# Output rows of a DMA-bound kernel: GpSimd's queue and its two row DMAs taken out, their rows put on SP

## The chip, the cores and the metric

The kernel runs on one core of one Trainium2 chip. Time is device microseconds of one execution, a median over several. The core has five engines: PE (TensorE), DVE (VectorE), ACT (ScalarE), POOL (GpSimd) and SP (SyncE), and 16 DMA engines that move data between HBM and the on-chip memory.
## The reference

Linear attention, then a soft mixture of experts, in float32:

```python
kv  = einsum('bhsd,bhse->bhde', k, v)                 # batch 8, heads 8, seq 576, dim 64
out = einsum('bhsd,bhde->bhse', q, kv)
x   = out / sqrt(mean(out*out, -1) + 1e-6) * g_norm   # -> 4608 tokens x 512
logits = x @ phi                                      # 4608 x 32 slots, 8 experts x 4 slots
d   = softmax of logits over the tokens               # 4608 x 32
slot_input = d.T @ x                                  # 32 x 512
slot_out[e] = relu(slot_input[e] @ w1[e]) @ w2[e]     # w1 8 x 512 x 1024, w2 8 x 1024 x 512
c   = softmax of logits over the slots
y   = c @ slot_out                                    # 4608 x 512
```

Read are q, k, v and the two weight tensors, 61.9 MB; written is y, 9.4 MB.

## The kernel before, in words

All large arrays pass through one on-chip buffer, `arena`, of 128 partitions (rows). SP issues nearly every transfer, and the order of its instructions is the order in which the DMA engines get work: first q, k and v by batch, then the weights in the rows of `W_ROWS`, each load as soon as its place in the arena is free, and at the end the output. The kernel keeps its own list of operations (`Order`), works out the waits of each from what it reads and writes (`settle`), and issues them at one line (`emit`, line 214, the waits at 213); this is why all rows of the profile have line 214. After the last operation SP waits at line 227 for every DMA that nobody has waited for.

The computation runs in stages of two token tiles (products, squares, root, logits, running maxima and sums), then the experts (`expert_h`, `expert_y`), and last the output. The output is made in 12 chunks, n = 0 to 11. A chunk is 128 rows of `CHUNK` = 1536 floats (6 KB a row, 768 KB in all). `output(hf, k, f)` makes chunk n: four matmuls, one ACT copy and one DVE copy from PSUM into the arena. Chunks 0 to 5 belong to the first half of the columns (hf = 0), 6 to 11 to the second; between the two PE has the rest of `expert_y` for the second half.

Chunks 3 to 11 are stored with three DMAs of all 128 rows by SP: chunks (3,4,5), (6,7) and (8,9,10,11) (`OUT_ROWS`), each issued once its last chunk has been copied. A DMA over 128 rows gives each DMA engine the same 8 rows.

Chunks 0, 1 and 2 are stored otherwise, by `store_first(n)`, which walks the list `FIRST`. Each entry is one DMA: an issuing engine, the first row `p0`, the step between rows, the number of rows `n`, the size `a` of the outermost dimension of the destination, the number of parts `c` into which each row is cut, and the chunks `k0` to `k1` that it takes of every row. It is issued after chunk `k1 - 1`:

```python
FIRST = (
    ("sync", 1, 4, 30, 5, 1, 0, 1), ("sync", 121, 4, 2, 3, 3, 0, 1),
    ("gpsimd", 1, 4, 24, 2, 1, 1, 2), ("gpsimd", 97, 4, 8, 2, 1, 1, 2),
    ("sync", 3, 4, 32, 1, 1, 0, 2), ("sync", 0, 2, 64, 1, 1, 0, 3), ("sync", 1, 2, 64, 1, 1, 2, 3),
)
STEPS = (7, 6)
```

The destination is written as `a` groups, and piece number j goes to group j mod a. So 30 rows with a = 5 go in five groups of six rows. `first_pieces` undoes this order on the host. `step_over(m)` issues a DMA of m tiny pieces from POOL, which carries nothing that is used (16 bytes per piece, from an input to the tile `stepped`). It is called once ahead of the experts with 7, and once between the two GpSimd entries of `FIRST` with 6.

Of the kernel before, what the change touches and what calls it, by code (L numbers as in the profile page):

```python
# [5 lines left out]
F32 = mybir.dt.float32  # L6
# [5 lines left out]
P = 128  # L12
# [41 lines left out]
OUT_ROWS = ((0, 1, 2), (3, 4, 5), (6, 7), (8, 9, 10, 11))  # L54
CHUNK = 4 * 12 * 32
FIRST = (
    ("sync", 1, 4, 30, 5, 1, 0, 1), ("sync", 121, 4, 2, 3, 3, 0, 1),
    ("gpsimd", 1, 4, 24, 2, 1, 1, 2), ("gpsimd", 97, 4, 8, 2, 1, 1, 2),
    ("sync", 3, 4, 32, 1, 1, 0, 2), ("sync", 0, 2, 64, 1, 1, 0, 3), ("sync", 1, 2, 64, 1, 1, 2, 3),
)  # L60
STEPS = (7, 6)
SHARED = (5, 11)
HEAD = 144
SCRATCH = 1024
# [210 lines left out]
def first_pieces(out):  # L275

    at = 0
    for _, p0, step, n, a, c, k0, k1 in FIRST:
        size = (k1 - k0) * CHUNK
        part = out[at : at + n * size]  # L280
        rows = part.reshape(n * c // a, a, size // c).swapaxes(0, 1)
        yield p0, step, n, k0, k1, rows.reshape(n, size)
        at += n * size

def soft_moe_linear_attention(nc, first_in, kv_in, q0_in, q1_in, kv4_in, kv5_in, t3_in, w_in, out):

    const = Const(nc)
# [9 lines left out]
    def place(at, n):  # L299
        return arena[:, HEAD + at * KB : HEAD + at * KB + n]  # L300
# [64 lines left out]
    nc.gpsimd.memset(ones, 1.0)  # L365
    zeros = const.tile([P, 256], BF16, name="zeros")
    nc.vector.memset(zeros, 0.0)
    stepped = const.tile([P, 16], F32, name="stepped")
    small = const.tile([P, 4], F32, name="small")
    eps = small[:, :1]  # L370
    nc.gpsimd.memset(eps, EPS_RMS)
# [304 lines left out]
    ends = {starts[s + 1] - 1: s for s in range(len(STAGES))}  # L676
# [194 lines left out]
    def expert_h(e):  # L871
        ph = ps.tile([P, 2, 512], F32, tag="m", name=f"ph{e}")[:, 0, :256]
        for c in range(4):
            for j in range(4):
                nc.tensor.matmul(
                    ph[32 * j : 32 * j + 32],
                    lhsT=sTe[:, (4 * e + c) * NS : (4 * e + c + 1) * NS],
                    rhs=w_block("w1", e, 4 * c + j),
                    start=c == 0,
                    stop=c == 3,  # L880
                )
        h = wk.tile([P, 256], F32, tag="part", name=f"h{e}", bufs=3)
        nc.scalar.activation(h, ph, AF.Relu, scale=rs)

        x = xts[(NT - 1 - e // 2) % NX].rearrange("p j n -> p (j n)")
        hTs[e] = x[:, e % 2 * 256 : e % 2 * 256 + 256].rearrange("p (c n) -> p c n", n=NS)
        nc.vector.transpose(out=hTs[e].rearrange("p c n -> p (c n)"), in_=h)
# [31 lines left out]
            nc.tensor.matmul(pz[f], lhsT=sel.rearrange("p a n -> p (a n)"), rhs=ys[hf][f], start=True, stop=True)  # L919
        zs[hf] = halves(f"z{hf}", pz)  # L920

    def step_over(n):
        ends = [x[:n, : 2 * w].rearrange("p (c n) -> p c n", c=2)[:, :, :4] for x, w in ((stepped, 8), (first_in, 64))]
        nc.gpsimd.dma_start(*ends)

    steps = list(STEPS[::-1])

    def store_first(n):
        at = 0
        for engine, p0, step, m, a, c, k0, k1 in FIRST:  # L930
            size = (k1 - k0) * CHUNK
            if k1 == n + 1:
                src = place(OUT_AT[k0], size)[p0 : p0 + step * (m - 1) + 1 : step]
                dst = out[:, at : at + m * size]
                if c > 1:
                    src = src.rearrange("p (c n) -> p c n", c=c)
                dst = dst.rearrange("o (b a n) -> (o a) b n", a=a, n=size // c)
                getattr(nc, engine).dma_start(dst, src)
                if engine == "gpsimd" and steps:
                    step_over(steps.pop())  # L940
            at += m * size

    def output(hf, k, f):
# [29 lines left out]
        if n <= OUT_ROWS[0][-1]:  # L973
            store_first(n)
        for row in OUT_ROWS[1:]:
            if row[-1] == n:
# [2 lines left out]
                    out[:, lo * P : (lo + m) * P].rearrange("o (p n) -> (o p) n", p=P), place(OUT_AT[row[0]], m)  # L979
                )  # L980

    step_over(steps.pop())
    expert_h(0)
    load_w("w2", 3)
    expert_h(1)
# [33 lines left out]
def build_program():  # L1019
    import concourse.bacc as bacc  # L1020

    nc = bacc.Bacc("TRN2", target_bir_lowering=False, num_devices=1, dynamic_dma_scratch_size=SCRATCH)
    shapes = {
        "first": (P, HEAD + 2304), "kv": (4, P, TOK), "q0": (P, TOK), "q1": (P, 2048),
        "kv4": (P, 2560 + TOK), "kv5": (P, 2 * TOK), "t3": (P, 3 * TOK),
        "w": (1, 2 * NE * P * UNIT),
    }
    args = [nc.dram_tensor(f"in_{n}_dram", s, F32, kind="ExternalInput").ap() for n, s in shapes.items()]
    args.append(nc.dram_tensor("out_0_dram", (1, 4 * NCH * P * 4 * CT * NS), F32, kind="ExternalOutput").ap())
    order = Order(nc)  # L1030
    soft_moe_linear_attention(order, *args)
    order.emit()
    return nc
# [61 lines left out]
```

How the kernel before makes its waits and increments, by code:

```python
    def emit(self):  # L203
        nc = self.nc
        counters = {e: nc.alloc_semaphore(f"done_{e}") for e in ENGINES[:4]}
        sems = list(counters.values())
        counts = dict.fromkeys(counters, 0)
        for op in self.ops:
            method, args, kwargs = op.call
            engine = getattr(nc, op.engine)
            *before, last = sorted(op.waits, key=lambda w: w.i) or [None]
            for w in before:
                engine.wait_ge(w.sem, w.value)
            inst = getattr(engine, method)(*args, **kwargs)
            if last is not None:
                inst.wait_op(last.sem, last.value, "sem-ge")
            if op.dma:
                op.sem, op.value = nc.alloc_semaphore(f"dma_{op.i}"), 16
                sems.append(op.sem)
                inst.then_inc(op.sem, 16)
            elif op.signals:
                counts[op.engine] += 1
                op.sem, op.value = counters[op.engine], counts[op.engine]
                inst.then_inc(op.sem, 1)
        for op in self.ops:
            if op.dma and not op.signals:
                nc.sync.wait_ge(op.sem, 16)
        numbers = sorted(s.num for s in sems)
        assert numbers == list(range(numbers[0], numbers[-1] + 1))
        nc.sync.sem_clear(range(numbers[0], numbers[-1] + 1))
```

## Time and profile before

| What | Value |
|---|---|
| time, median of 3 runs (lowest, highest) | 172.08 us (171.82 to 172.19) |
| profiled execution, its own time | 171.97 us |
| its span, first to last instruction | 170.6 us |
| bytes moved by the DMA engines | 71.65 MB, mean 420 GB/s |
| busy share of the span: PE, PEld, DVE, ACT, POOL | 87%, 62%, 51%, 52%, 35% |
| DMA packets: SP's queue (q1), GpSimd's queue (q0) | 3994, 352 |

The page cuts the span into 40 slices; its row DMA gives the mean busy share of the 16 DMA engines in tenths, its row GB/s what they moved. The view of DMA queues gives the same for any stretch, with the packets that start in it.
### The profile page before, as it was taken

What the parts mean: (1) busy time and instruction counts of PE and PEld (TensorE: products, weight loads), DVE (VectorE), ACT (ScalarE), POOL (GpSimd) and SP (SyncE); (2) the same over time, 40 slices, a digit from 0 to 9 for tenths busy, and PEclk for the clock granted to TensorE, in tenths of its full rate; (3) what the DMA queues carried; (4) which work ended last, traced back from release to release, by engine and by line L of the source; (5) the groups of instructions that cost most, each with busy time, mean ns of one, the idle gap of its engine ahead of it and who ended that gap; (6) DMA issues with size and microseconds to landing.
All of it is one profiled execution on the core that took longest, in us unless ns stands there. A gap on an engine that the chain in (4) does not pass through costs nothing.

```text
span 170.6 us, 4233 instructions
## 1 busy us (share of the span) xinstructions
PE 149.0 (87%) x1832; PEld 105.0 (62%) x1832; DVE 86.6 (51%) x185; ACT 89.0 (52%) x230; POOL 59.6 (35%) x73
## 2 busy tenths in 40 slices
PE   7989696989999899999899998989999989989300
PEld 3468576979778888897697674346655543455000
DVE  1122156284677266762946698823888137218400
ACT  3027576796975886859759864202223045217400
POOL 7000707648357745377382679500000004000000
PEclk9999999999999999999999999999999999999955
DMA  5999999999999999999999999999999999999996
GB/s 186 417 429 421 444 415 439 473 416 452 462 415 421 432 441 430 419 399 451 415 449 407 455 392 421 447 434 415 430 426 442 436 442 392 431 419 434 416 455 277
DMA packets 4365, 71.65 MB, mean 420 GB/s; under 512 B 790, under 2 KB 790, under 8 KB 922
## 3 DMA queue, kind: packets, MB, share of 16 engines
q1 hardware_dynamic: 3994, 71.18, 97.8%
q8 instruction: 14, 0.23, 0.5%
q0 software_dynamic: 352, 0.20, 0.4%
q14 instruction: 5, 0.04, 0.1%
HBM read 61.94 MB, written 9.44 MB: 418 GB/s over the span
## 4 chain that ended last, share of the span: by engine, by line
PE 58%; DMA 13%; ACT 12%; DVE 7%; SPq 2%; issue 1%
PE psum L214 58%; DMA arena<-in_kv_dram 13%; ACT bd L214 3%; ACT sq L214 3%; ACT xall L214 2%; SPq L214 2%; DVE arena L214 1%; DVE logits L214 1%; ACT arena L214 1%; DVE ms L214 1%; ACT part L214 1%; ACT d L214 1%; DVE part L214 1%; ACT r L214 1%; DVE acc L214 1%
## 5 line engine op out<-in xcount | busy, mean ns | idle before, releaser
L214 PE MATMUL psum<-bd,arena 128*128 128x192 f32 (+1 forms) x320 | 56.1, 335 | 1.9 <-ACT bd L214 1.5
L214 PEld LDWEIGHTS psum<-bd,arena 128*128 128x128 f32 (+1 forms) x320 | 45.4, 179 | 8.7 <-ACT bd L214 2.8
L214 DVE TENSOR_REDUCE ms<-sq 128x16 f32<-128x1024 f32 (+1 forms) x19 | 22.1, 1162 | 32.8 <-ACT sq L214 32.5
L214 POOL TENSOR_TENSOR part<-part,r 128x512 f32<-128x512 f32 x17 | 17.8, 1048 | 49.6 <-DVE r L214 49.6
L214 POOL TENSOR_TENSOR xall<-xall,r 128x512 f32<-128x512 f32 x34 | 34.7, 1042 | 0.0
L214 ACT ACTIVATE sq<-psum 128x512 f32<-128x512 f32 x36 | 21.5, 598 | 11.7 <-PE psum L214 11.2
L214 PE MATMUL psum<-arena 128*64 128x64 f32 (+1 forms) x640 | 21.7, 226 | 2.8 <-DMA arena<-in_kv_dram 2.7
L214 PEld LDWEIGHTS psum<-arena 128*64 128x64 f32 (+1 forms) x640 | 19.0, 137 | 8.2 <-DMA arena<-in_kv_dram 3.6
L214 ACT COPY xall<-psum 128x512 f32<-128x512 f32 x34 | 20.6, 606 | 0.0
L214 ACT COPY part<-psum 128x256 f32<-128x256 f32 (+1 forms) x38 | 13.6, 359 | 11.2 <-DVE part L214 10.0
L214 DVE TENSOR_REDUCE logits<-part 128x64 f32<-128x512 f32 (+1 forms) x18 | 17.8, 988 | 0.0
L214 PE MATMUL psum<-logits,part 32*128 32x384 f32 x96 | 13.5, 523 | 1.5 <-ACT arena L214 0.7
L214 PE MATMUL psum<-arena,xall 128*32 128x256 f32 x256 | 14.7, 380 | 0.0
L214 ACT COPY arena<-psum 128x768 f32<-128x768 f32 (+1 forms) x14 | 10.2, 754 | 5.3 <-PE psum L214 5.2
L214 POOL DMA_DIRECT2D out_dram<-arena x2 | 1.2, 589 | 33.4 <-ACT arena L214 33.4
L214 PE MATMUL psum<-arena,sq 128*32 128x256 f32 x224 | 12.7, 379 | 0.2 <-DVE sq L214 0.2
L214 DVE COPY arena<-psum 128x768 f32<-128x768 f32 (+1 forms) x12 | 10.3, 888 | 4.7 <-PE psum L214 4.7
L214 PEld LDWEIGHTS psum<-arena,xall 128*32 128x32 f32 x256 | 8.3, 110 | 6.0 <-issue 1.0
L214 PE MATMUL psum<-xall,d 128*32 128x258 f32 x144 | 10.8, 390 | 0.8 <-ACT d L214 0.8
L214 PEld LDWEIGHTS psum<-logits,part 32*128 32x128 f32 x96 | 6.3, 183 | 7.8 <-ACT arena L214 4.3
L214 ACT COPY bd<-psum 64x128 f32<-64x128 f32 (+1 forms) x32 | 9.9, 309 | 1.6 <-PE psum L214 1.4
L214 PEld LDWEIGHTS psum<-arena,sq 128*32 128x32 f32 x224 | 7.2, 110 | 5.1 <-DVE sq L214 0.5
(80 smaller groups left out, 124.1 us busy)
## 6 DMA issues: line engine op xcount, KB each, us to landing
arena<-in_w_dram SPq DMA_DIRECT2D x4, 4096.0 KB, 23.5
arena<-in_w_dram SPq DMA_DIRECT2D x4, 2048.0 KB, 20.0
arena<-in_t_dram SPq DMA_DIRECT2D x1, 6912.0 KB, 36.1
arena<-in_w_dram SPq DMA_DIRECT2D x2, 3072.0 KB, 22.6
arena<-in_kv_dram SPq DMA_DIRECT2D x2, 2304.0 KB, 23.6
arena<-in_kv_dram SPq DMA_DIRECT2D x1, 4608.0 KB, 42.8
arena<-in_kv_dram SPq DMA_DIRECT2D x1, 3584.0 KB, 32.4
arena<-in_kv_dram SPq DMA_DIRECT2D x3, 1152.0 KB, 12.0
```

Of the source, the lines that this page charges most:

```text
L214: inst = getattr(engine, method)(*args, **kwargs)
```

## The change

`FIRST` loses the column of the issuing engine: all entries are issued by SP. The two GpSimd entries, which stored rows 1, 5, 9, ... of chunk 1, are gone, and so are `step_over`, `STEPS` and the tile `stepped`. Those rows of chunk 1 now go with the last entry, which takes all odd rows of chunks 1 and 2 (it took chunk 2's alone). Rows 3, 7, ... are now stored for chunk 0 alone in their entry (before: chunks 0 and 1), and that entry is issued after chunk 0. Rows 1, 5, ... of chunk 0 are split anew: 25 rows in five groups, and 7 rows, each cut in two parts, in two groups. The number of SP's store DMAs stays five for these chunks.

```diff
 FIRST = (
-    ("sync", 1, 4, 30, 5, 1, 0, 1), ("sync", 121, 4, 2, 3, 3, 0, 1),
-    ("gpsimd", 1, 4, 24, 2, 1, 1, 2), ("gpsimd", 97, 4, 8, 2, 1, 1, 2),
-    ("sync", 3, 4, 32, 1, 1, 0, 2), ("sync", 0, 2, 64, 1, 1, 0, 3), ("sync", 1, 2, 64, 1, 1, 2, 3),
+    (1, 4, 25, 5, 1, 0, 1), (101, 4, 7, 2, 2, 0, 1), (3, 4, 32, 1, 1, 0, 1),
+    (0, 2, 64, 1, 1, 0, 3), (1, 2, 64, 1, 1, 1, 3),
 )
-STEPS = (7, 6)
...
-    stepped = const.tile([P, 16], F32, name="stepped")
...
-    def step_over(n):
-        ends = [x[:n, : 2 * w].rearrange("p (c n) -> p c n", c=2)[:, :, :4] for x, w in ((stepped, 8), (first_in, 64))]
-        nc.gpsimd.dma_start(*ends)
-
-    steps = list(STEPS[::-1])
-
     def store_first(n):
         at = 0
-        for engine, p0, step, m, a, c, k0, k1 in FIRST:
+        for p0, step, m, a, c, k0, k1 in FIRST:
...
-                getattr(nc, engine).dma_start(dst, src)
-                if engine == "gpsimd" and steps:
-                    step_over(steps.pop())
+                nc.sync.dma_start(dst, src)
...
-    step_over(steps.pop())
     expert_h(0)
```

## Rows read from the trace of the kernel before

**Rows 1.** The page: DMA busy share and rate in 40 slices, and the queues.
```profile
DMA  5999999999999999999999999999999999999996
GB/s 186 417 429 421 444 415 439 473 416 452 462 415 421 432 441 430 419 399 451 415 449 407 455 392 421 447 434 415 430 426 442 436 442 392 431 419 434 416 455 277
...
q1 hardware_dynamic: 3994, 71.18, 97.8%
...
q0 software_dynamic: 352, 0.20, 0.4%
```

**Rows 2.** Windows: busy time of each engine, PE's clock, DMA share and GB/s.
```profile
20.00:136.00 116.00, 110.85 (x1418) 82.68 (x1422) 71.14 (x156) 70.27 (x194) 52.68 (x54) 1.00 1.01 431
136.00:146.00 10.00, 8.66 (x70) 4.15 (x60) 5.59 (x8) 5.23 (x8) 1.72 (x3) 1.00 0.99 420
146.00:158.00 12.00, 11.26 (x144) 6.38 (x145) 4.31 (x7) 4.17 (x8) 0.00 (x0) 1.00 1.01 421
```

**Rows 3.** Timeline from 159 us on: start, duration, instruction.
```profile
159.68 0.48 ACT L214 COPY arena<-psum 128x384 f32<-128x384 f32 x1 [0.34 <-PE psum L214]
160.27 0.33 SPq L214 DMA_DIRECT2D out_dram<-arena  x1
```

**Rows 4.** SP's waits from 136 us on: in total, times, longest.
```profile
SPq L227 <- DMA out_dram<-arena: 9.6, 2, 7.2
```

**Rows 5.** DMA queues, 168.4 to 169.2 us: packets that start there, by size.
```profile
DMA packets 15, 0.25 MB, mean 307 GB/s; under 512 B 5, under 2 KB 5, under 8 KB 5
```

**Rows 6.** DMA queues, 169.2 to 169.8 us.
```profile
DMA packets 2, 0.02 MB, mean 41 GB/s; under 512 B 1, under 2 KB 1, under 8 KB 1
```

**Rows 7.** 169.8 to 170.0 and 170.0 to 170.2 us: 40 slices of 5 ns.
```profile
GB/s 0 1 0 0 0 1 0 0 0 0 0 0 0 0 0 0 0 0 0 0 0 0 0 0 0 0 0 0 0 0 0 0 1 0 0 0 0 1 1 0
DMA packets 5, 0.00 MB, mean 0 GB/s; under 512 B 5, under 2 KB 5, under 8 KB 5
...
GB/s 0 0 0 0 0 0 1 0 0 0 0 1 0 0 1 0 1 0 0 0 0 0 0 0 0 1 0 0 0 0 0 0 0 0 0 0 0 0 0 0
```

**Rows 8.** DMA queues, 146 to 158 us: packets, MB, share of the 16 engines.
```profile
DMA packets 733, 5.06 MB, mean 421 GB/s; under 512 B 356, under 2 KB 356, under 8 KB 486
...
q1 hardware_dynamic: 415, 4.84, 95.1%
q0 software_dynamic: 317, 0.20, 5.6%
```

**Rows 9.** DMA queues, 143.5 to 145.6 us, and 145.6 to 146.0 us.
```profile
DMA packets 56, 0.84 MB, mean 398 GB/s; under 512 B 5, under 2 KB 5, under 8 KB 5
...
DMA packets 19, 0.22 MB, mean 553 GB/s; under 512 B 4, under 2 KB 4, under 8 KB 6
```

**Rows 10.** Instructions that store the output, 138-142, 142-144, 143-145 and 145-161 us.
```profile
L214 SPq DMA_DIRECT2D out_dram<-arena x3: 530/722/951, 140.2 to 142.0; - x3
...
L214 POOL DMA_DIRECT2D out_dram<-arena x2: 569/589/609, 142.2 to 143.4; - x2
...
L214 SPq DMA_DIRECT2D out_dram<-arena x2: 502/546/589, 142.8 to 143.3; - x2
...
L214 SPq DMA_DIRECT2D out_dram<-arena x3: 332/344/358, 147.2 to 160.3; - x3
```

**Rows 11.** The page's DMA issues: count, KB each, us from issue to landing.
```profile
out_dram<-arena SPq DMA_DIRECT2D x1, 3072.0 KB, 10.2
...
out_dram<-arena SPq DMA_DIRECT2D x2, 384.0 KB, 9.7
out_dram<-arena POOLq DMA_DIRECT2D x1, 144.0 KB, 11.9
out_dram<-arena POOLq DMA_DIRECT2D x1, 48.0 KB, 15.4
```

More of the change, by code:

```diff
@@ L277, in first_pieces @@
     at = 0
-    for _, p0, step, n, a, c, k0, k1 in FIRST:
+    for p0, step, n, a, c, k0, k1 in FIRST:
         size = (k1 - k0) * CHUNK
```

## The prediction

> **What bounds the kernel now.** I read the page first, its DMA rows before its engines. The 16 DMA engines are full in every slice but the first and the last, and SP's queue alone fills 97.8% of them [rows 1]. The windows say the same: 431 GB/s from 20 to 136 us, 420 and 421 in the two stretches behind [rows 2]. PE is busy too, but it isn't what ends last: the last copy starts at 159.68 us, SP issues the last store at 160.27 [rows 3], and from there to the end no compute engine does anything, while SP waits for stores, 9.6 us in two waits [rows 4]. The last store has 3072 KB and lands 10.2 us after its issue [rows 11], at 160.27 + 10.2 = 170.5 of a span of 170.6. At 431 GB/s it would need 7.3 us by itself, so it stands behind other work: the DMA engines are behind the computation by some 3 us. The computation could be earlier or a little later and the end would not move. What sets the end is the DMA engine with the most to carry, and how evenly the bytes lie over the 16.
>
> Then I cut the end into narrow windows and counted the 4-byte packets, one per DMA engine, with which the last store ends. Five engines close it before 169.2 us [rows 5], one between 169.2 and 169.8 [rows 6], five in 169.8 to 170.0 and five in 170.0 to 170.2 [rows 7]. A slice there is 5 ns, and the 1s are the packets: the first of these ten is at 169.805 us, the third at 169.96, the last at 170.125 (SP sees it some 0.35 us later). So ten of 16 engines end within 0.32 us, and the other six up to 1.7 us earlier. Any change that leaves the sum of bytes alone can gain only what those six have spare; it loses as soon as one of the last ten gets more.
>
> **The change part by part.** One DMA engine carries 431 / 16 = 26.9 GB/s [rows 2], so 6 KB (one row of one chunk) is 0.228 us and 12 KB is 0.456 us.
>
> *Which engine gets what.* The bytes that move are rows 1, 5, ... of chunks 0 and 1, 384 KB. I deal them out by the code: a piece goes to group j mod a, and I take a group for one DMA engine.
>
> Before: 36 KB to each of engines 0 to 4 (30 rows in five groups); two more rows, 12 KB, which I take for engine 0, since the source has 2 rows and the destination 3 groups, with no count in common; over GpSimd 72 KB to each of two engines (24 rows in two groups) and 24 KB to each of two (8 rows). The counts 7, 2, 6, 2 of GpSimd's four DMAs add up to 17, one more than 16; if they are dealt in turn from engine 0, the pairs are 7 and 8, and 15 and 0. Engine 0 then has 36 + 12 + 24 = 72 KB, engines 1 to 4 have 36, 7 and 8 have 72, 15 has 24, and eight engines have nothing: 72 + 144 + 144 + 24 = 384.
>
> After: 30 KB to each of engines 0 to 4 (25 rows), 42 KB to engine 0 (7 rows against 2 groups, again no common count), and chunk 1's rows spread evenly, 12 KB each. Engine 0 has 84, engines 1 to 4 have 42, the other eleven 12: 84 + 168 + 132 = 384.
>
> The difference: +12 KB (+0.456 us) for nine engines (0 and the eight that had nothing), +6 KB (+0.228) for four, -12 KB for one, -60 KB (2.3 us) for two. The two will end early, and nothing uses their time.
>
> *What the nine do to the end.* Only six engines close before 169.8 us [rows 5, 6]. So at least three of the nine are among the last ten, which gives a new end no earlier than that of the third of the ten. The lower bound is therefore 169.96 + 0.456 = 170.42, 0.29 us behind 170.125 [rows 7], the upper one 0.456 us. Nine engines out of 16 will nearly always hold one of the last five, so I take the upper end, +0.45. If GpSimd's pairs lie elsewhere, at least 16 - 5 - 4 = 7 engines have nothing before and 12 KB after, against six early ones: the argument stands.
>
> The Trainium skill (DMA: Bandwidth & Descriptors, "Why a DMA increments its semaphore by 16 and not by 1") says that the engines used are the largest number up to 16 that divides the slowest dimension of both sides, the lowest-numbered from SP, and in turn from GpSimd; by that rule the shares are as I dealt them. No row of before names a DMA engine.
>
> *GpSimd's queue goes away.* From 146 to 158 us its 317 packets take 5.6% of the 16 engines [rows 8], 0.67 us on each. The 192 KB that it carried are 12 KB per engine, 0.456 us, and are still carried by SP's queue. The rest, 0.67 - 0.456 = 0.21 us per engine, is some 285 tiny packets, 18 per engine, and is saved. Outside the packets the queue might slow the others. The bound above: the rate is 421 GB/s there against 431 before, over 12 us that is 0.28 us in all; but it is 420 from 136 to 146 [rows 2], where that queue carries nothing yet (its first two packets start behind 145.6 us, as do the first rows of 6 KB [rows 9]), so I count the packets' 0.21 alone. The bound below is nothing, if other tiny packets take their place.
>
> *Smaller pieces.* Engine 0 gets 14 pieces of 3 KB for six of 2 KB. A tiny packet costs 0.21 / 18 = 12 ns, so eight more are at most 0.1 us, on that engine alone. I count nothing, since the other eight set the same end.
>
> *Issues on SP.* It issues five DMAs for these chunks before and after, 502 to 951 ns each [rows 10]. One moves from chunk 1 to chunk 0, GpSimd's two vanish, and chunk 1's rows now wait for chunk 2. The last issue of before starts at 143.3 us [rows 10], and the first row of 6 KB leaves behind 145.6 [rows 9]. So every store of these chunks is in the queue some 2 us before an engine comes to it, and the order costs nothing. Without that cover each late issue would cost its 0.5 us. Behind them SP has nothing until 147.2 [rows 10]. POOL has nothing to do there, and the two tiny copies signal nobody. The two engines that lose 60 KB come to the last store 2.3 us earlier, at about its issue; a wait there costs nothing, since they have that time spare.
>
> *Sum.* +0.45 - 0.21 = +0.24 us on the profiled execution's 171.97, so 172.21. The median shown is 0.11 above that execution, so 172.08 + 0.24 = **172.32 us**, 0.14% slower. Differences below 0.2%, 0.34 us, are about what a measurement of this kernel can't tell from nothing. The case's own range goes from +0.29 - 0.28 to +0.46, and 0.1 for engine 0: 172.09 to 172.64.
>
> **The rivals.**
>
> *Engine 0 is overloaded (slower).* If GpSimd's second pair does not hold engine 0, this engine goes from 48 to 84 KB: 36 KB, 1.37 us. Should it be one of the last ten, the end moves by 1.37 - 0.21 = 1.16 us, to 173.2. If instead the two-group DMA does use two engines, 21 KB each, engines 0 and 1 go from about 40 to 63 KB, 0.87 us, and the end by 0.66, to 172.7. For it: nothing in the entries evens engine 0 out. Against it: before, engine 0 has 48 KB from SP alone and may be one of the six early ones. It decides if engine 0 ends now after 170.12 + 0.45 - 1.37 = 169.2 us.
>
> *The two terms cancel (no change).* The last engines are mainly the four with +0.23, and the saving is 0.28: -0.05 to 0, 172.1. For it: the bounds above. Against it: then three of the nine at most are late.
>
> *GpSimd's queue costs more than its packets (faster).* Its descriptors are written and fetched beside the traffic, and its set-up may lie in the 1.37 us outside the span. To come out faster by more than 0.34 us it would have to cost 0.45 + 0.34 = 0.8 us. For it: 11.9 and 15.4 us from issue to landing against 9.7 for SP's stores of 384 KB [rows 11], though more bytes per engine explain that. Against it: the rate with and without that queue, 421 and 420. I give it 171.6. The Trainium skill (DMA: Bandwidth & Descriptors, "Latency and other measured facts") has its best guess that fetching GpSimd's descriptors slows engines 7 and 15; by that rule the removal would gain on these two. The trace agrees with no such loss in its rates, and those two have time spare after the change.
>
> **How the numbers follow.** My forecast's case 0.50, engine 0 overloaded 0.20, cancelled 0.16, faster 0.12, anything else 0.02. The range takes in the forecast's case and the cancelled one whole, the two-engine form of the overload and a part of the faster case: 171.8 to 172.8. Faster by over 0.2%: 0.13. Within: two thirds of 0.50, 0.16, and a little of the overload, 0.51. Slower: the upper part of the forecast's case, 172.42 and above, and most of the overload, 0.36.
>
> **What would show it.** q0 is gone from the list of queues, and SP's packets carry 71.4 MB. The last store's 16 closing packets: two some 2.3 us before the old ones, near 167.7; the last ones 0.25 us later than before. The last store is issued at 160.3 as before, and lands after 10.4 us. The computation is unchanged up to 160.3. I am wrong if one engine stands alone at the end (the overload), if the last closing packets come earlier than 170.1 us of the span, or if the time outside the span moves by more than 0.2 us.

## The result, and the profile after

The changed kernel took 172.31 us (median of 20 runs, 172.22 to 172.72) where the kernel before took 172.01 (20 runs on the same chip, 171.82 to 172.43). The ratio is 1.0019, its 95% interval 1.0013 to 1.0025: 0.33 us slower, between 0.22 and 0.43 (the two medians alone differ by 0.30). A single execution of each of two kernels below took 789.40 and 215.16 us, and the ratios leave these two out. A second series of the unchanged text of the changed kernel gave 172.30 and 1.0016 (1.0007 to 1.0025). The forecast was 172.32. The profiled execution took 172.27 us with a span of 170.9; before they were 171.97 and 170.6. Outside the span the two have the same 1.37 us by these rounded numbers.

The page after, its DMA rows, to be laid beside [rows 1]:

```profile
DMA  5999999999999999999999999999999989999995
GB/s 188 426 426 428 435 422 436 473 415 473 431 418 425 444 440 430 399 408 449 422 441 445 406 435 410 441 433 410 433 426 437 473 380 429 425 429 428 411 451 236
DMA packets 4016, 71.65 MB, mean 419 GB/s; under 512 B 470, under 2 KB 470, under 8 KB 541
...
q1 hardware_dynamic: 3997, 71.38, 97.9%
q8 instruction: 14, 0.23, 0.5%
q14 instruction: 5, 0.04, 0.1%
```

q0 is gone, the bytes are the same, the DMA engines are full as before, and the last slice has less in it (236 for 277 GB/s): the end is more uneven. The same windows as [rows 2], and the queues from 146 to 158 us beside [rows 8]:

```profile
20.00:136.00 116.00, 110.81 (x1418) 82.65 (x1422) 71.20 (x156) 70.11 (x194) 51.89 (x53) 1.00 1.01 431
136.00:146.00 10.00, 8.66 (x71) 4.13 (x64) 5.52 (x8) 5.23 (x8) 0.00 (x0) 1.00 0.99 424
146.00:158.00 12.00, 11.26 (x144) 6.46 (x145) 4.31 (x7) 4.10 (x8) 0.00 (x0) 1.00 1.00 423
```

```profile
DMA packets 424, 5.07 MB, mean 423 GB/s; under 512 B 73, under 2 KB 73, under 8 KB 142
...
q1 hardware_dynamic: 423, 5.06, 99.2%
```

From 146 to 158 us there are 73 packets under 512 bytes instead of 356, and the rate is 423 GB/s for 421, too little to read a gain from. The end, beside [rows 3], [rows 4] and [rows 11], from the timeline, SP's waits and the DMA issues:

```profile
159.71 0.56 DVE L212 COPY arena<-psum 128x384 f32<-128x384 f32 x1 [0.46 <-PE psum L212]
...
160.34 0.33 SPq L212 DMA_DIRECT2D out_dram<-arena  x1
```

```profile
SPq L225 <- DMA out_dram<-arena: 9.9, 2, 7.2
```

```profile
out_dram<-arena SPq DMA_DIRECT2D x1, 3072.0 KB, 10.4
```

The last store is issued at 160.34 us (before 160.27) and lands 10.4 us later (10.2). SP's waits grow from 9.6 to 9.9 us. So the computation is where it was, and the 0.3 us lie in how the last store lands. Its closing packets, in the windows of [rows 5, 6, 7] and two more behind them (a slice of the GB/s rows is 5 ns):

```profile
DMA packets 14, 0.17 MB, mean 215 GB/s; under 512 B 7, under 2 KB 7, under 8 KB 7
...
DMA packets 9, 0.20 MB, mean 328 GB/s; under 512 B 1, under 2 KB 1, under 8 KB 1
...
DMA packets 0, 0.00 MB, mean 0 GB/s; under 512 B 0, under 2 KB 0, under 8 KB 0
...
GB/s 0 0 0 0 0 0 0 0 0 0 0 0 0 0 0 0 0 0 0 0 0 0 0 1 0 0 0 0 0 0 0 0 0 0 0 0 0 0 0 0
...
GB/s 1 0 0 1 0 0 1 0 1 0 0 0 0 0 1 0 0 0 0 1 0 0 0 0 0 0 0 0 0 0 0 0 0 0 0 0 0 0 0 0
...
GB/s 0 0 1 0 0 0 0 0 0 0 0 0 0 0 0 0 0 0 0 0 0 0 0 0 0 0 0 0 0 0 0 0 0 0 0 0 0 0 0 0
```

Closings per window, before and after: 168.4 to 169.2 us five and seven; to 169.8 one and one; to 170.0 five and none; to 170.2 five and one; to 170.4 none and six; behind that none and one, at 170.41. So the early group has two more, as it must if the two DMA engines that lost 60 KB were late ones, the late group has eight for ten, and its last closing is at 170.41 instead of 170.125, 0.285 us later. That is nearly all of the span's 0.3.

So the packets can be strung into 16 lists. Where an engine had nothing to do its list breaks, and there two engines can be mistaken for each other. That is so for most early ones, which stood idle for 0.3 to 0.6 us at about 157.1 us and again at 161.2, waiting for a store. Of the eight late ones of the changed kernel, seven have lists that run through. From 146 us on the lists show this:

- In the changed kernel five rows of 6 KB and then 14 pieces of 3 KB lie on one engine, as the prediction dealt them to engine 0. It closes at 170.295 us, 0.12 ahead of the last one; in the profile of the second series it closes at 169.997, the first of the eight late ones.
- In the kernel before, the engine with the pieces of 2 KB also carries four of GpSimd's 32 rows, the 24 KB that the prediction dealt to it, and it closes last, at 170.125 us. The other 28 fit twelve, twelve and four.
- Five engines end their last weight load at 148.8 to 149.0 us, the other eleven at 145.9 to 147.7. These five close at 170.20 to 170.41 us. The other three of the late eight are engine 0 and two of engines 1 to 4. So most late engines are late since the weight loads, before any output is stored.

### The profile page after: what moved, and what is told of

Same layout as the page of the kernel before. It is cut to its first block, busy times and chain, and to the rows that moved or that the text cites. A ratio compares the mean times of both kernels' runs of the same rounds, so it can differ in the third digit from the quotient of the medians.

```text
span 170.9 us, 4226 instructions
## 1 busy us (share of the span) xinstructions
PE 149.2 (87%) x1832; PEld 105.0 (61%) x1832; DVE 86.6 (51%) x185; ACT 89.0 (52%) x230; POOL 57.2 (33%) x69
## 3 DMA queue, kind: packets, MB, share of 16 engines
q1 hardware_dynamic: 3997, 71.38, 97.9%
## 4 chain that ended last, share of the span: by engine, by line
PE 48%; DMA 23%; ACT 12%; DVE 7%; SPq 2%; issue 1%
PE psum L212 48%; DMA arena<-in_kv_dram 13%; DMA arena<-in_w_dram 10%; ACT bd L212 3%; ACT sq L212 3%; ACT xall L212 2%; SPq L212 2%; DVE arena L212 1%; DVE logits L212 1%; ACT arena L212 1%; DVE ms L212 1%; ACT part L212 1%; ACT d L212 1%; DVE part L212 1%; ACT r L212 1%
## 5 line engine op out<-in xcount | busy, mean ns | idle before, releaser
L212 ACT COPY part<-psum 128x256 f32<-128x256 f32 (+1 forms) x38 | 13.6, 359 | 11.4 <-DVE part L212 10.2
L212 ACT COPY arena<-psum 128x768 f32<-128x768 f32 (+1 forms) x14 | 10.2, 754 | 5.3 <-PE psum L212 5.2
L212 ACT ACTIVATE r<-ms,small 128x16 f32<-128x16 f32 x17 | 5.2, 308 | 5.9 <-DVE ms L212 5.9
```

Of the source, the lines that this page charges most:

```text
L212: inst = getattr(engine, method)(*args, **kwargs)
```

## The experiments

Ten kernels ran, and the changed kernel once more. All times of "before" below are runs of that kernel on the same chip beside the kernel named. A tiny packet is one under 512 bytes.

**Even chunk 1 alone: does engine 0's load or chunk 0's new split matter?** The changed kernel with chunk 0's rows 1, 5, ... split as before, so engine 0 has 24 KB less than in the changed kernel:

```diff
-    (1, 4, 25, 5, 1, 0, 1), (101, 4, 7, 2, 2, 0, 1), (3, 4, 32, 1, 1, 0, 1),
+    (1, 4, 30, 5, 1, 0, 1), (121, 4, 2, 3, 3, 0, 1), (3, 4, 32, 1, 1, 0, 1),
```

> GpSimd's rows spread evenly over SP, chunk 0's rows dealt as before (48 KB on engine 0, 36 KB on engines 1 to 4). My theory, that the fullest DMA engine sets the end: the eight engines that had nothing get 12 KB as in the changed kernel, so 0.456 - 0.21 = +0.25 us against before, the same as the changed kernel (+0.30 measured) within 0.1; engines 1 to 4 get 12 KB more, no more than the others. Rival, engine 0 (84 KB) sets the changed kernel's end: here it has 60 KB, 24 KB less, and the end would come 0.2 us or more ahead of the changed kernel's, at before's time or below it.

Measured: 172.31 us against 172.11; 1.0016 (1.0007 to 1.0025), as the changed kernel. Neither engine 0's 24 KB nor the smaller pieces decide; the whole difference to before is made by chunk 1's rows and the queue that they left. It was close for engine 0: with its 84 KB it closes 0.12 us ahead of the last one.

**All of it even: what does another 12 KB on the late engines cost?** The changed kernel with chunk 0's odd rows spread like the rest: 12 KB more for DMA engines 5 to 15, less for 0 to 4.

```diff
-    (1, 4, 25, 5, 1, 0, 1), (101, 4, 7, 2, 2, 0, 1), (3, 4, 32, 1, 1, 0, 1),
-    (0, 2, 64, 1, 1, 0, 3), (1, 2, 64, 1, 1, 1, 3),
+    (0, 2, 64, 1, 1, 0, 3), (1, 2, 64, 1, 1, 0, 3),
```

> All rows of chunks 0 to 2 spread evenly, 24 KB of the moved rows on each engine. My theory: the eight engines that had nothing get 24 KB, 0.91 - 0.21 = +0.70 us against before, 0.45 more than in the changed kernel. Rival, the queue that issues or the number of SP's issues decides, and not the place of the bytes: two store DMAs for these chunks in place of five, so no slower than the changed kernel, +0.3 us or less.

Measured: 172.70 us (172.64 to 172.72) against 172.11; 1.0038 (1.0025 to 1.005). On the same chip the kernel with even chunk 1 had 172.31, so 12 KB more cost 0.39 us, of 0.456 by the rate. Its closings, in windows 169.8:170, 170:170.2, 170.2:170.6 and 170.6:170.8:

```profile
DMA packets 5, 0.05 MB, mean 246 GB/s; under 512 B 3, under 2 KB 3, under 8 KB 3
...
DMA packets 7, 0.00 MB, mean 0 GB/s; under 512 B 7, under 2 KB 7, under 8 KB 7
...
DMA packets 1, 0.00 MB, mean 0 GB/s; under 512 B 1, under 2 KB 1, under 8 KB 1
...
GB/s 0 0 0 0 0 0 0 0 0 0 1 1 0 1 0 0 0 0 0 0 0 0 0 0 0 1 0 0 0 0 0 0 0 1 0 0 0 0 0 0
```

The last closing is at 170.765 us, 0.355 behind the changed kernel's. This profile is disturbed in another place, and the windows show it (column PEclk, the third from the end):

```profile
146.00:148.00 2.00, 2.00 (x18) 0.81 (x20) 0.07 (x1) 0.48 (x1) 0.00 (x0) 0.67 0.99 426
148.00:150.00 2.00, 2.00 (x24) 1.09 (x20) 0.00 (x0) 0.00 (x0) 0.00 (x0) 0.50 0.98 419
150.00:152.00 2.00, 2.00 (x43) 1.17 (x36) 0.00 (x0) 0.00 (x0) 0.00 (x0) 0.98 1.02 433
...
161.87 0.33 SPq L211 DMA_DIRECT2D out_dram<-arena  x1
```

From about 147 to 150 us PE worked at a granted clock of 0.50, its 1.2 GHz level. Ahead of that it had done the same as in the changed kernel, to 0.01 us in each stretch of matmuls (3.58 us, 0.2 idle, 0.91 us), where the clock stayed at 1.00; why it fell here no row tells. The last store was issued 1.5 us later than in the changed kernel. The first ten closings are those of DMA engines that had run out of work and waited for this store: they come between 169.99 and 170.13 us, 8.12 to 8.26 us after its issue. The six behind them had older work still, and they set the end. So even 1.5 us of computation was hidden for the engines that decide.

**No steps: does the fullest engine set the end?** The kernel before without the tiny DMAs, so that its rows are dealt to other DMA engines:

```diff
-                if engine == "gpsimd" and steps:
-                    step_over(steps.pop())
-    step_over(steps.pop())
```

> The kernel before without its two tiny GpSimd copies, so that GpSimd's two row DMAs are dealt from the first engine on. My theory: the pairs are then engines 0 and 1 (72 KB each) and 2 and 3 (24 KB each). Engine 0 goes from 72 to 120 KB, +1.82 us, engine 1 from 36 to 108, +2.7 us; the end moves by +1.8 to +2.7 us. Rival, the DMA engines take GpSimd's rows wherever there is room, or in other places than I dealt them: no change, within 0.2 us.

Measured: 174.25 us against 172.11; 1.0127 (1.0113 to 1.0141), 2.14 us slower with the same bytes on the same queues. Its closings, in windows 169:170, 170:170.4, 170.4:171.2, 171.2:172.2 and 172.2:173:

```profile
DMA packets 16, 0.25 MB, mean 246 GB/s; under 512 B 6, under 2 KB 6, under 8 KB 6
...
DMA packets 2, 0.00 MB, mean 0 GB/s; under 512 B 2, under 2 KB 2, under 8 KB 2
...
DMA packets 3, 0.05 MB, mean 61 GB/s; under 512 B 1, under 2 KB 1, under 8 KB 1
...
DMA packets 2, 0.02 MB, mean 25 GB/s; under 512 B 1, under 2 KB 1, under 8 KB 1
...
DMA packets 1, 0.00 MB, mean 0 GB/s; under 512 B 1, under 2 KB 1, under 8 KB 1
```

Three DMA engines stand alone, the last of them, at 172.475 us, 2.35 behind the thirteenth: this is what an overloaded one looks like, and the changed kernel shows nothing of it. It also bears out the dealing that the prediction took: without the two tiny DMAs GpSimd's 24 rows begin at engine 0, which already has 48 KB. Strung together, twelve GpSimd rows lie on the engine with the pieces of 2 KB (it closes at 171.765 us) and twelve on one of engines 1 to 4 (172.475), and two more of engines 1 to 4 have four each (170.887 and 169.882). The Trainium skill (DMA: Bandwidth & Descriptors, "Why a DMA increments its semaphore by 16 and not by 1") has GpSimd's DMAs in turn over consecutive engines; this run agrees, for the tiny DMAs carry nothing and move the time by 2.14 us.

**GpSimd's rows spread over all engines: bytes or queue?** The kernel before, GpSimd keeping its queue and its 192 KB, dealt evenly:

```diff
-    ("gpsimd", 1, 4, 24, 2, 1, 1, 2), ("gpsimd", 97, 4, 8, 2, 1, 1, 2),
+    ("gpsimd", 1, 4, 16, 1, 1, 1, 2), ("gpsimd", 65, 4, 16, 1, 1, 1, 2),
```

> The kernel before, with GpSimd's 32 rows of chunk 1 in two DMAs of 16 rows that use all 16 engines (12 KB on each); the two tiny copies stay. The bytes of each DMA engine are those of e1_chunk1_even, only the queue differs. My theory, the queue costs its tiny packets, some 20 per engine at 9 to 12 ns: 0.18 to 0.24 us above e1_chunk1_even, so +0.4 to +0.45 us against before. Rival, GpSimd's queue costs nothing: as e1_chunk1_even, +0.20. Rival, it costs more than its packets: +0.7 or more.

Measured: 172.36 us against 172.13; 1.0015 (1.0006 to 1.0024). That is the time of the kernel with even chunk 1, which has the same 12 KB per engine on SP's queue (1.0016). So, to within the 0.2 us that two such series can tell apart, the queue that carries the bytes does not matter, and the place does. The +0.4 to +0.45 expected did not come, and neither did the 20 tiny packets per engine that it was reckoned from. There are 96 in all, 6 per engine, as the page and the window 146:158 show:

```profile
q0 software_dynamic: 128, 0.20, 0.3%
```

```profile
q1 hardware_dynamic: 420, 4.87, 95.6%
q0 software_dynamic: 96, 0.20, 4.3%
```

**What do GpSimd's tiny packets cost?** Three kernels put a GpSimd queue back into the changed kernel. The first has four tiny DMAs of the old step's form (7, and behind it in POOL's order 12, 6 and 4):

```diff
+        if n == 1:
+            for m in (12, 6, 4):
+                step_over(m)
...
+    step_over(7)
```

> The changed kernel with four GpSimd DMAs put back that carry next to nothing (7, 12, 6 and 4 rows of two 16-byte pieces into a tile that nobody reads), one ahead of the experts, three after chunk 1; the output's rows are dealt as in the changed kernel. My theory, each tiny packet costs some 12 ns on its DMA engine and nothing else: between +0.1 and +0.21 us against the changed kernel, so +0.4 to +0.5 against before. Rival, the queue costs nothing that shows: as the changed kernel, +0.30. Rival, it costs more than its packets: +0.8 or more.

Measured: 172.38 us against 172.11; 1.002 (1.001 to 1.0029). The second gives two of the four the two-group form of the old row DMAs, with 16-byte pieces for rows:

```diff
+    def tiny(n, at):
+        nc.gpsimd.dma_start(stepped[:n, at : at + 4], first_in[:n, :4].rearrange("(b a) n -> a b n", a=2))
...
+        if n == 1:
+            tiny(24, 4)
+            step_over(6)
+            tiny(8, 12)
```

> The changed kernel with four GpSimd DMAs put back in the shapes that they had before (7 rows, 24 rows dealt in two groups, 6 rows, 8 rows in two groups), but with 16 bytes per piece in place of 6 KB, into a tile that nobody reads. The first trial of this kind brought only 128 tiny packets against 320 before, so it could not price them all. If the groups of two bring them back (some 320), my sum has them at 0.21 us: +0.5 us against before, 0.2 above the changed kernel. Rival, tiny packets fit between the others and cost nothing, and what the changed kernel loses is only its 12 KB, less than 0.456 us as the last engines differ: +0.30, as the changed kernel.

Measured: 172.50 us against 172.17; 1.0019 (1.001 to 1.0028). Both pages say `q0 software_dynamic: 128, 0.00, 0.0%` where I wanted the 352 of before. These two can't show the price of 320 tiny packets, and they miss the place too: the tiny DMAs wait for no store, and POOL issued them between 107.9 and 127.2 us in the first kernel and between 108.0 and 115.9 in the second, beside weight loads. With ratios of 1.002 and 1.0019 beside the changed kernel's 1.0019 they show no cost of 128, to some 0.2 us; both expectations' +0.4 to +0.5 were missed. The third has real rows of 3 KB in the two-group form, written to places that the last store overwrites later, 96 KB more than the reference needs:

```diff
+        dst = out[:, at : at + n * 768].rearrange("o (b a n) -> (o a) b n", a=2, n=768)
+        nc.gpsimd.dma_start(dst, place(OUT_AT[1], 768)[lo : lo + n])
...
+            to_two(24, 0)
+            step_over(7, 32)
+            step_over(7, 64)
+            to_two(8, 32)
```

> The changed kernel with five GpSimd DMAs put back (7 tiny rows, 24 rows in two groups, twice 7 tiny rows, 8 rows in two groups), now as stores of 3 KB a row after chunk 1, at the time that they had before. They write to rows of the output that the last store overwrites, and that store waits for them as well. 36 and 12 KB fall on each of two engines, 7 and 8 by the counts, which have 2 us to spare. So the queue is back in place and time, and no late engine gets its bytes. Tiny packets at 9 ns each: +0.1 to +0.2 us above the changed kernel, +0.4 to +0.5 against before. Rival, the tiny packets cost nothing: +0.3, as the changed kernel. Rival, a second queue slows every packet beside it, as it did beside the weight loads in e9_loads_for_two: +0.8 or more.

Measured: 172.45 us against 172.03; 1.0025 (1.0015 to 1.0035), 0.1 to 0.15 us more than the changed kernel in its two series. Here POOL issued the row DMAs at 141.3 and 143.0 us, the place of before (142.2 and 143.4). Its page, and its window 146:158:

```profile
q0 software_dynamic: 256, 0.10, 0.2%
```

```profile
DMA packets 621, 5.13 MB, mean 427 GB/s; under 512 B 258, under 2 KB 258, under 8 KB 342
...
q1 hardware_dynamic: 420, 5.02, 98.6%
q0 software_dynamic: 200, 0.09, 2.6%
```

The 32 rows of 3 KB went as 16 packets of 6 KB (so the packed trace), which leaves 240 tiny ones. At 0.21 us for 285 they would cost 0.18. The 0.1 has an interval of about 0.2 either way: it agrees with the packets' price and with half of it, and speaks against the rival's queue, which asked for 0.5 more than the changed kernel.

**GpSimd's loads in that place.** The same with loads of 3 KB rows from an input for the stores, into a part of the arena that is free:

```diff
+    def to_two(n, lo):
+        src = first_in[lo : lo + n, :768].rearrange("(b a) n -> a b n", a=2)
+        nc.gpsimd.dma_start(place(40, 768)[lo : lo + n], src)
```

> The changed kernel with four GpSimd DMAs put back: 7 tiny rows, 24 rows dealt in two groups, 14 tiny rows, 8 rows in two groups. The row DMAs load 3 KB per row into a place that is free by then and that nobody reads, 36 and 12 KB on each of two engines; by the counts both pairs are engines 7 and 8, which lost 60 KB by the change and have 2 us to spare at the end. So the queue is back with real rows, and no late engine gets a byte of them. If that brings the tiny packets back (320 before), my sum has them at 0.21 us: +0.2 above the changed kernel on the same chip, +0.5 against before. Rival, they cost nothing: as the changed kernel, +0.3. If the two groups lay elsewhere, 48 KB on a late engine would show as +1.8 us or more.

Measured: 173.42 us against 171.99; 1.008 (1.0067 to 1.0092), 1.4 us: far more than the sum had, and short of the 1.8 for rows on a late engine. Nor does one engine stand alone: the last nine closings lie between 170.757 and 171.535 us. The loads wait for nothing that the stores wait for, and the timeline shows them issued at 127 us, beside SP's weight loads. The windows 130:146 of this kernel and of the changed one stand below, and a count of the queues of this one:

```profile
126.92 0.62 POOL L212 DMA_DIRECT2D arena<-in_first_dram  x1 [18.26 <-PE psum L212]
127.52 0.55 POOL L212 DMA_DIRECT2D stepped<-in_first_dram  x1
128.07 0.58 POOL L212 DMA_DIRECT2D arena<-in_first_dram  x1
...
130.00:146.00 16.00, 14.23 (x174) 7.30 (x162) 7.95 (x15) 5.72 (x10) 0.00 (x0) 1.00 1.00 403
...
q1 hardware_dynamic: 289, 6.31, 97.1%
q0 software_dynamic: 192, 0.10, 2.1%
```

```profile
130.00:146.00 16.00, 14.45 (x175) 7.51 (x167) 8.19 (x15) 5.78 (x10) 0.00 (x0) 1.00 1.01 430
```

The rate falls from 430 to 403 GB/s with the DMA engines as busy as before: (430 - 403) / 430 x 16 us = 1.0 us lost, most of the 1.1 by which this kernel is behind the changed one on the same chip (172.30). SP's own packets are slower: a load packet of 32 KB takes 1321 ns (median, 134 to 138 us), and 1213 in the changed kernel. This run tells nothing of the old stores, which came later; it shows that the same queue can cost beside loads what its packets' time doesn't explain (2.1% of 16 us are 0.34). Why, no run here tells.

**Can a better balance beat both?** Six DMA engines of the kernel before close up to 1.54 us ahead of the last (the first at 168.58 us). I tried to give 15 more rows (90 KB, three groups) to engines which I took for early, over GpSimd, and to spread the rest of those rows over all 16. One of these 17, written as 16 parts, went as a single packet of 6 KB all the same:

```diff
+    ("gpsimd", 3, 4, 15, 3, 1, 1, 2),
+    ("sync", 63, 4, 1, 16, 16, 1, 2), ("sync", 67, 4, 16, 1, 1, 1, 2),
...
-STEPS = (7, 6)
+STEPS = (7, 6, 12)
```

> The kernel before, and of chunk 1's rows 3, 7, ... only 17 still spread evenly (6.4 KB per engine in place of 12); the other 15 go over GpSimd in three groups, dealt after a further tiny copy of 12 rows, so to engines 13 to 15 if the dealing is in turn (30 KB each). My theory, the end is the fullest DMA engine's, and engines 13 to 15 end early: all the late ones lose 5.6 KB, 0.21 us, two more GpSimd DMAs with some ten tiny packets per engine cost 0.09 at most, so -0.1 to -0.2 us against before; engines 13 to 15 gain 24.4 KB, 0.93 us, and stay behind the late ones. Rival, engines 13 and 14 are themselves among the late ones: +0.9 us. Rival, more GpSimd DMAs cost more than the evenness gives: +0.1 or more.

Measured: 172.86 us against 172.17; 1.0042 (1.0028 to 1.0055), a loss where I expected a gain. Its closings, in windows 168:169.8, 169.8:170.4 and 170.4:171:

```profile
DMA packets 27, 0.49 MB, mean 273 GB/s; under 512 B 7, under 2 KB 7, under 8 KB 7
...
DMA packets 9, 0.05 MB, mean 82 GB/s; under 512 B 7, under 2 KB 7, under 8 KB 7
...
DMA packets 2, 0.00 MB, mean 0 GB/s; under 512 B 2, under 2 KB 2, under 8 KB 2
```

Fourteen close by 170.4 us and two stand alone behind: two of the three engines that got the rows were not early. The next run has two steps of 6 for the one of 12, in case it was the step that dealt them otherwise than I took:

```diff
-STEPS = (7, 6, 12)
+STEPS = (7, 6, 6, 6)
```

> As e5b_three_more, where two DMA engines ended 0.9 us behind the rest, but the tiny copy of 12 rows ahead of the third row DMA is two of 6 rows. If a DMA of 12 rows does not move the dealing on by 12 (it may be dealt over 16), the 15 rows lay on engines 1 to 3 there, and lie on 13 to 15 only here. My theory with 13 and 14 early: all the late engines lose 5.6 KB, 0.21 us, less some tiny packets, so -0.1 to -0.2 us against before. Rival, the dealing was as counted and 13 and 14 are among the late ones: +0.7 as before. In both cases the fullest engine sets the end; a result near before's, with no engine apart at the end, would speak against it.

Measured: 173.04 us (172.84 to 173.5) against 172.11; 1.0053 (1.004 to 1.0067). Again a loss. Both agree with the rule that the fullest late engine sets the end. Where the rows went, the packets of this second kernel tell, strung together. The two engines that close last, at 170.982 and 171.586 us, carry five GpSimd rows each, between 156.8 and 161.1 us, where both lists run through without a break. A third engine carries nine, the four of the old DMA and five more, which by the counts makes it engine 15; it closes early, at 169.196. So the dealing was as counted, on engines 13, 14 and 15, and the rival was right: 13 and 14 are late ones. The list of the one leads back to a weight load that ended at 148.9 us or at 148.7; the other's has a break of 0.2 us at 154.3. No version faster than the kernel before was found.

**The changed kernel once more**, to see how far two series of one kernel differ:

> The changed kernel as it is, beside the run before it on the same chip: +0.3 us against before by both theories.

Measured: 172.30 us against 171.99; 1.0016 (1.0007 to 1.0025).

## Why the prediction was right, point by point

**The end is the DMA engines', not the computation's: right.** The last store was issued at 160.34 us, as before, and all of the 0.3 us is in its landing. The all-even kernel issued it 1.5 us later, and only those engines felt it that had nothing else to do.

**The fullest late engines set the end, and the place of the bytes counts: right, and shown.** Same bytes, 64 packets fewer, other engines: 2.14 us (no steps), with the rows found on the engines that the dealing names. Same bytes per engine on another queue: no difference (1.0015 and 1.0016). Another 12 KB on the late ones: 0.39 us.

**+0.45 us for nine engines: right in kind, a little high if anything.** The next 12 KB cost 0.39 us by the medians and 0.355 by the last closing of one profile (0.31 if it is set beside the closing of even chunk 1, 170.46), against 0.456 by the rate. The late group shifted as a whole, eight closings of ten from around 170.0 to around 170.3.

**-0.21 us for GpSimd's tiny packets: the right sign, too large; the traces have 0.12.** A tiny packet takes 9 ns in the packed trace, and the next one on its engine starts 3 ns ahead of its end: three in a row start at 147.185, 147.191 and 147.197 us. So it holds its engine for 6 ns, where the prediction had 12. The 320 of before are 20 per engine, 0.12 us. The prediction took the price from the queue's time, 0.67 us per engine [rows 8], less 0.456 for the rows. But the rows took 0.51 of it, since three of them needed 356, 448 and 593 ns in place of 234, and the tiny packets only 0.16 at 9 ns each. With 0.12 the sum is +0.456 - 0.12 = +0.34 us, and +0.33 was measured (0.22 to 0.43), or +0.30 in the profiled executions.

The runs by themselves are too coarse for this term. From before to even chunk 1 (12 KB more, queue gone) is +0.20 us by the medians and 0.28 by the ratio; from there to all even (12 KB more, nothing else) is +0.39 and 0.38. If both 12 KB cost the same, the queue's going gave 0.19 us, or 0.10. Set against the rate's 0.456 it is 0.26, or 0.18. Adding 240 tiny packets beside stores cost 0.1 to 0.15, where 6 ns each give 0.09. All of these have an uncertainty of 0.1 to 0.2.

**The time itself: luck.** 172.32 was forecast and 172.31 measured. The forecast stood on 172.08 for the kernel before, which 20 runs then put at 172.01, and its difference of 0.24 was short by 0.06 to 0.09.

**Small pieces, SP's issues: nothing, right.** With the old split of chunk 0 the time is the same, and the last issue is where it was.

**The signs to look for.** q0 gone, 71.38 MB on SP's queue, last store issued at 160.3 and landed after 10.4 us, last closing 0.25 later (it was 0.285): right. One was wrong: two closings near 167.7 us. I worked them out as the old ones less 2.3 us, and forgot that an engine can't close the last store before it has carried its share of it. The two went where the store's own issue put them: in this kernel no closing comes before 168.4 us,

```profile
DMA packets 17, 0.42 MB, mean 418 GB/s; under 512 B 0, under 2 KB 0, under 8 KB 0
```

(window 167.4:168.4), and the first is at 168.47, 8.13 us behind the issue at 160.34; the waiting engines of the all-even kernel came 8.12 us behind theirs. The working had said that their wait costs nothing, which holds; only the sign was placed wrongly. It also follows that the closing of an engine that waited doesn't show all of its spare time: the prediction's "up to 1.7 us earlier" counts from the closings alone.

**The rivals.** *Engine 0 overloaded* falls: no closing stands alone, and 24 KB less on that engine change nothing. Its condition doesn't hold either: the engine had four GpSimd rows before and so gained 12 KB, not 36. But it is one of the last, before and after, against the prediction's guess that it might be an early one. *The terms cancel* falls with the interval's lower end, +0.22 us. *GpSimd's queue costs more than its packets* falls for this place, by the sum itself and by the kernel with 256 packets put back. It would have been right beside loads: there 192 packets went with 1.0 us. The Trainium skill's guess (DMA: Bandwidth & Descriptors, "Latency and other measured facts") that engines 7 and 15 suffer from GpSimd's queue finds nothing here: by the dealing engine 15 is the one with nine GpSimd rows in the kernel with two steps of 6, and it is among the early ones. Beside the loads the rate of all 16 together fell by 6%, which two engines alone would have to pay with half of theirs (27 of 2 x 26.9 GB/s).

**What stays open**: why five DMA engines end the weight loads 1 to 3 us behind the others with equal shares of nearly everything.

## What to carry to other kernels

In a kernel bound by its DMA engines, look at the closing packets of the last transfer before you move any bytes: they tell how many engines are late, how much spare the others have at least, and hence what any redistribution can gain and what it can lose. An even split is not free when the load is already uneven: 12 KB on each of the late engines cost what they cost, 0.4 us, whichever queue brings them. And spare time is of use only on engines that are known to have it: two well-meant tries on engines that I took for early lost 0.7 and 0.9 us. Strung together by their starts, the packets of before would have warned of it: of the eight engines that carry none of the moved rows there, 13 and 14 among them by the dealing, five are late.

## What was not expected of the hardware

**Tiny packets depend on the form of a GpSimd DMA.** q0 had 352 packets before for 32 rows, 288 without the two tiny DMAs, and 128 when the same rows went in two DMAs of 16 rows over all engines. So each row DMA in two groups brought (288 - 32) / 2 = 128 packets beside its rows, each in the all-engine form (128 - 64 - 32) / 2 = 16, and each step 32. With 16-byte pieces in place of the rows the two-group form did not bring them, and with rows of 3 KB each brought 72: (240 - 3 x 32) / 2. The page of the kernel without steps:

```profile
q0 software_dynamic: 288, 0.20, 0.4%
```

**A second queue's loads beside large loads slow all engines**: 430 to 403 GB/s for 0.1 MB in 192 packets, while stores of the same form beside SP's stores left the rate alone (427 from 146 to 158 us, where the changed kernel has 423).

**From issue to closing there is a floor**: an engine that waits for a store of 3072 KB closes it 8.12 to 8.13 us behind SP's issue, of which its share at 26.9 GB/s is 7.3. The other 0.8 is the start: the first packets of these stores leave 0.84 us (changed kernel, 161.18) and 0.83 us (all even, 162.70) behind the issue.

**A tiny packet holds its DMA engine for 6 ns**, 9 ns long less the 3 ns by which the next one starts ahead of its end.
